# Second gate's products from three bfloat16 parts, two routings begun before a block end, and a rearranged last overflow tile in a fused attention and mixture-of-experts kernel

## What is computed

```python
def _moe_ref(x, w_skip, w_gate, w1, w2):          # first mixture
    do_compute = x @ w_skip > 0
    out = x.copy()
    xc = x[do_compute]
    logits = xc @ w_gate
    e_idx = np.argmax(logits, axis=1)
    gate_w = softmax(logits)[np.arange(len(xc)), e_idx]
    for e in range(E):
        mask = e_idx == e
        h = np.maximum(xc[mask] @ w1[e], 0.0)
        y[mask] = gate_w[mask, None] * (h @ w2[e])
    out[do_compute] = xc + y

def _moe2_ref(x, w_gate, w1, w2):                 # second mixture
    logits = x @ w_gate
    # (token, expert) pairs in falling order of their logit; a token goes to
    # the first expert that has room, and each expert takes N // E = 384
    for e in range(E):
        mask = assigned == e
        out[mask] = np.maximum(x[mask] @ w1[e], 0.0) @ w2[e]
```

## Time and profile before

| what | us |
|---|---|
| median of 3 runs | 808.35 |
| lowest and highest | 808.31, 808.92 |
| the profiled execution, whole | 809.03 |
| its span, first to last instruction | 807.3 |
| PE, DVE, ACT, POOL busy | 752.7, 536.9, 453.4, 165.3 |

### The profile page before, as it was taken

The page is one execution under the profiler, slowest core; times in us unless marked ns, Lnnn a source line. Parts: engine busy times, 40 slices in busy tenths (PEclk is TensorE's granted clock), DMA queues, the critical chain, the costliest instruction groups (busy, mean ns, idle before and its releaser), DMA issues. The chain is left out here.

```text
span 807.3 us, 15740 instructions
## 1 busy us (share of the span) xinstructions
PE 752.7 (93%) x5588; PEld 676.4 (84%) x5590; DVE 536.9 (67%) x1463; ACT 453.4 (56%) x919; POOL 165.3 (20%) x184
## 2 busy tenths in 40 slices
PE   2899999999869999999999929999999999999997
PEld 2899999999738998899988816888888888888895
DVE  6877878778388768775566557666676767675420
ACT  3899999989425545465454304555545454636360
POOL 8100000000030322213221101141414142323221
PEclk9999999999979999999999957999999999999999
DMA  8999989986265457634663007868676777769861
GB/s 180 218 214 251 227 195 251 217 227 177 107 180 196 156 216 250 217 129 165 228 233 122 18 2 248 201 198 202 204 188 209 186 220 187 220 180 303 225 126 44
DMA packets 64106, 151.65 MB, mean 188 GB/s; under 512 B 12294, under 2 KB 15750, under 8 KB 64016
## 3 DMA queue, kind: packets, MB, share of 16 engines
q1 hardware_dynamic: 52512, 114.77, 48.6%
q0 software_dynamic: 11504, 35.72, 18.3%
HBM read 118.84 MB, written 16.67 MB: 168 GB/s over the span
## 5 line engine op out<-in xcount | busy, mean ns | idle before, releaser
L1817 PE MATMUL r_ph<-r_xh,r_w1h 128*128 128x384 f32 x256 | 90.7, 354 | 0.0
L1817 PE MATMUL r_ph<-r_xh,r_w1l 128*128 128x384 f32 x256 | 86.2, 337 | 0.0
L1817 PE MATMUL r_ph<-r_xl,r_w1h 128*128 128x384 f32 x256 | 85.8, 335 | 0.0
L592 ACT ACTIVATE pr<-pr,nmx 128x232 f32<-128x232 f32 (+1 forms) x192 | 79.9, 467 | 4.1 <-DVE nmx L685 2.6
L1098 PE MATMUL m_ph<-m_xh,m_w1h 128*128 128x224 f32 x288 | 81.0, 281 | 0.1
L1252 ACT ACTIVATE m_hh<-m_ph 128x224 fp32r<-128x224 f32 (+1 forms) x72 | 25.1, 349 | 98.0 <-PE m_ph L1098 94.1
L1098 PE MATMUL m_ph<-m_xh,m_w1l 128*128 128x224 f32 x288 | 79.1, 275 | 0.0
L1098 PE MATMUL m_ph<-m_xl,m_w1h 128*128 128x224 f32 x288 | 79.0, 274 | 0.0
L685 DVE CUSTOM_DVE_ANT_0 pr<-sc,bias 128x232 f32<-128x232 f32 (+1 forms) x192 | 65.1, 375 | 19.4 <-PE sc L466 16.4
L599 ACT ACTIVATE prt<-tp 128x384 f32<-128x384 f32 (+1 forms) x128 | 65.3, 535 | 20.4 <-PE tp L478 17.0
L1831 PE MATMUL r_py<-r_w2h,r_hh 128*128 128x512 f32 x192 | 76.1, 397 | 0.0
(11 more groups left out here) (298 smaller groups left out, 1960.7 us busy)
## 6 DMA issues: line engine op xcount, KB each, us to landing
r_w<-moe_w SPq DMA_DIRECT2D x64, 512.0 KB, 5.1
m_w<-moe_w SPq DMA_DIRECT2D x36, 512.0 KB, 5.6
row_buf<-moe_w SPq DMA_DIRECT2D x9, 2048.0 KB, 8.7
r_w2l<-r_w POOLq DMA_DIRECT2D x32, 512.0 KB, 4.9
k_raw<-kI SPq DMA_DIRECT2D x64, 208.0 KB, 7.2
q_raw<-qT SPq DMA_DIRECT2D x64, 192.0 KB, 8.2
vo<-vL SPq DMA_DIRECT2D x16, 384.0 KB
x_rows<-row_buf SPq DMA_DIRECT2D x4, 1536.0 KB, 6.6
```

The lines of the kernel that those rows point to most:

```text
L592: nc.scalar.activation(pr[n % PRS][:, t, lo:CW], pr[n % PRS][:, t, lo:CW], ACT.Exp, bias=nmx[n % PRS][:, t:t + 1], scale=-1.0).then_inc(ex ...
L1817: last = nc.tensor.matmul(ph[m % 4][:, 0:CAP], w[:, c, m * P:(m + 1) * P], x[:, c, :], start=(c == 0 and a == 0), stop=(c == KC - 1 and a ...
```

## The change

1. **z of blocks 0 to 6 from bfloat16 parts.** ACT copies the transposed rows as bfloat16 (`y_parts[0]`), DVE subtracts that from the bank (`yt`), ACT takes the bfloat16 of the rest (`y_parts[1]`), DVE the rest of that (`y_parts[2]`). The gate's weights are split once, in `split_gate2`, four DVE operations put at the head of `count_extra`. The product takes each of the three parts of y with the 24 columns of the three parts of the gate: 24 bfloat16 products for a block instead of 8 float32 ones. DVE adds three columns for each logit (`tensor_reduce`) instead of copying. The z of block 7 and of overflow tiles stay in float32.
2. **Four steps instead of three**, behind chunks (1, 3, 4, 7), and (2, 3, 4, 5) in the overflow block. The product is the last step.
3. **`open_route`**: the first seven operations of `route` run on DVE at the end of the attention block, after `take_logits`. The semaphore `asked`, on which PE's counts waited, goes.
4. **Clearing**: `xg` is cleared by two ACT operations ahead of its w1 parts, not by POOL; POOL clears the ends of the three `y_parts` and waits for all six before it issues its first indirect DMA.
5. **`open_search`**: `bests`, `needs` and the first candidates (11 operations) run on DVE at the end of the first mixture's block.
6. **Overflow tile**: its four transposes go to four banks, without the wait for ACT between them. Four filler products follow the spreading of the marks, two follow the transpose of the limits.
7. **DVE's branches**: the code for n below 1 and over 1 comes before the code for n = 1, so that behind `put_z` none is left.

```diff
-BUSY1, BUSY2 = (18, 4, 3), (18, 4, 6)
+BUSY1, BUSY2, BUSY_END = (18, 4, 3), (18, 4, 6), (4, 2)
...
+                def open_route(link):
+                    by_expert = [P, E, NT]
+                    dve.wait_ge(filled, FILLS + 3)
+                    link(v.tensor_reduce(best1[:], logits[:, :, 0:E], AX.X, ALU.max))
+                    link(v.tensor_tensor(work1[:], logits[:, :, 0:E].rearrange("p t e -> p e t"), best1[:].unsqueeze(1).broadcast_to(by_expert), ALU.is_equal))
+                    link(v.tensor_scalar(live1[:], logits[:, :, E], 0.0, None, ALU.is_gt))
...
+                    link(v.tensor_tensor(hot1[:], work1[:], live1[:].unsqueeze(1).broadcast_to(by_expert), ALU.mult))
...
+                    dve.wait_ge(read, B)
+                    open_route(link)
...
-            Z_AT, OVER_AT = (2, 3, 5), 3
+            Z_AT, Z_LAST, OVER_AT = (1, 3, 4, 7), (2, 3, 4, 5), 3
...
+            def turned_rows(k, c):
+                return pt[c % 2][:, BLK:] if c < 2 or len(tiles(k)) == 2 else (py[1], ph[2])[c - 2][:, 0:P]
...
-                for s in range(2):
-                    g.memset(xg[s][:], 0.0).then_inc(cleared, 1)
                 g.memset(never[:], NO_ROW).then_inc(cleared, 1)
-                pool.wait_ge(cleared, 3)
+                for part in y_parts:
+                    g.memset(part[:, :, WIDE1:], 0.0).then_inc(cleared, 1)
+                pool.wait_ge(cleared, 6)
...
+                    elif i == 3 and in_parts(k):
+                        pe.wait_ge(yt_kept, kept_before(k) + 6)
+                        pe.wait_ge(yt_low, kept_before(k) + 6)
...
+                        for t in tiles(k):
+                            for c in range(KC):
+                                for a in range(3):
+                                    last = nc.tensor.matmul(pt[0][:, BLK + t * 3 * E:BLK + (t + 1) * 3 * E], y_parts[a][:, c, t * P:t * P + P],
+                                                            wg2_parts[:, c].rearrange("p a e -> p (a e)"), start=(c == 0 and a == 0), stop=(c == KC - 1 and a == 2))
+                        last.then_inc(z_done, 1)
...
-                pe.wait_ge(asked, 1)
...
                         nc.tensor.matmul(taken_p, spot_lane[:], spot_tile[:], start=True, stop=True).then_inc(taken_up, 1)
+                        keep_busy(BUSY_END[0], ph[3])
...
                         turn_limits()
-                    z_part(E, 0, 2)
+                        keep_busy(BUSY_END[1], ph[3])
+                    z_part(E, 0, 3)
...
+                    if i in (1, 2) and in_parts(k):
+                        two = slice(2 * i - 2, 2 * i)
+                        act.wait_ge(yt_low, kept_before(k) + 2 * i)
+                        nc.scalar.activation(y_parts[1][:, two, 0:WIDE1], yt[:, two, 0:WIDE1], ACT.Copy).then_inc(yt_kept, 1)
...
+                for s in range(2):
+                    nc.scalar.activation(xg[s][:].rearrange("p t d -> p (t d)"),
+                                         ones[:, 0:1].broadcast_to([P, TT1 * DM]), ACT.Copy, scale=0.0).then_inc(cleared, 1)
...
+                    if i < 2 and in_parts(k):
+                        for c in (2 * i, 2 * i + 1):
+                            dve.wait_ge(yt_kept, kept_before(k) + c + 1)
+                            v.tensor_tensor(yt[:, c, 0:WIDE1], pt[c % 2][:, BLK:BLK + WIDE1], y_parts[0][:, c, 0:WIDE1], ALU.subtract).then_inc(yt_low, 1)
+                    if i in (1, 2) and in_parts(k):
+                        two = slice(2 * i - 2, 2 * i)
+                        dve.wait_ge(yt_kept, kept_before(k) + 4 + i)
+                        v.tensor_tensor(y_parts[2][:, two, 0:WIDE1], yt[:, two, 0:WIDE1], y_parts[1][:, two, 0:WIDE1], ALU.subtract).then_inc(yt_low, 1)
...
+                def split_gate2():
+                    link(v.tensor_copy(wg2_parts[:, :, 0, :], wg2[:]))
+                    link(v.tensor_tensor(wg2_rest[:], wg2[:], wg2_parts[:, :, 0, :], ALU.subtract))
+                    link(v.tensor_copy(wg2_parts[:, :, 1, :], wg2_rest[:]))
+                    link(v.tensor_tensor(wg2_parts[:, :, 2, :], wg2_rest[:], wg2_parts[:, :, 1, :], ALU.subtract))
...
                 def count_extra():
+                    split_gate2()
...
+                with dve.If(n < 1):
+                    limits_of_all(Chain(dve, alone_chain))
+                with dve.If(n > 1):
...
                 with dve.If(n > 0):
-                    one_block(E, P)
                     with dve.If(n < 2):
+                        one_block(E, P)
...
                         put_z(alone)
+                        open_search(alone)
...
-                bests(logits2)
-                needs()
                 for r in range(TRIES):
                     attempt(0, r)
```

More of the change, by code:

```diff
@@ L804, in build @@
             yt = tb("yt", [P, KC, BLK])
+            y_parts = [tb(f"y_part{i}", [P, KC, BLK], BF16) for i in range(3)]
             zo = [tb(f"zo{s}", [P, TT1, E]) for s in range(2)]
@@ L1151, in over_table, with keep_busy @@
                     last.then_inc(over_placed, 1)
-                def keep_busy(times):
+                def keep_busy(times, bank=py[0]):
                     for i in range(times):
-                        nc.tensor.matmul(py[0][:], onesb1[:], busy[:, 0:512], start=True, stop=True)
-                pe.wait_ge(asked, 1)
+                        nc.tensor.matmul(bank[:], onesb1[:], busy[:, 0:512], start=True, stop=True)
                 flat = hot[:].rearrange("p e t -> p (e t)")
@@ L1277, in _ @@
                     one_block(E, P)
-                    for i in range(3):
+                    for i in range(4):
                         z_part(E, i)
@@ new lines, in limits_of_all, with more @@
+                def limits_of_all(alone):
+                    limit(alone)
+                    limit_all(alone)
+                    keep_limits(alone)
+                    open_search(alone)
+                def more(k):
+                    next_parts(k, 0, P)
+                    one_block(k, P)
+                    y_keep(k, 0)
+                    for i in range(4):
+                        z_part(k, 0, i)
+                with dve.If(n < 1):
+                    limits_of_all(Chain(dve, alone_chain))
@@ L1560, in _ @@
                         put_z(alone)
-                    with dve.If(n > 1):
-                        y_keep(E, 0)
-                        z_part(E, 0, 2)
-                def more(k):
-                    next_parts(k, 0, P)
-                    one_block(k, P)
-                    y_keep(k, 0)
-                    for i in range(3):
-                        z_part(k, 0, i)
-                further(dve, n, more)
-                for other in (n < 1, n > 1):
-                    with dve.If(other):
-                        alone = Chain(dve, alone_chain)
-                        limit(alone)
-                        limit_all(alone)
-                        keep_limits(alone)
+                        open_search(alone)
         late.close()
@@ L1607, in build @@
             masked, tie, ranks = (tb(x, shape) for x in ("masked", "tie", "ranks"))
-            work, hot, gt, taken = (tb(x, shape, BF16) for x in ("work", "hot", "over", "taken"))
+            work, hot, best, bestm, bestw, need, needc, scr8, span, candf = (
+                work2, hot2, best2, bestm2, bestw2, need2, needc2, scr2, span2, candf2)
+            gt, taken = (tb(x, shape, BF16) for x in ("over", "taken"))
             firstb = firstb1
-            best, bestm, cmp1, rank1, high = (tb(x, [P, NT]) for x in ("best", "bestm", "cmp1", "rank1", "high"))
-            bestw, cmpb, ours, mem, upto, low = (tb(x, [P, NT], BF16) for x in ("bestw", "cmpb", "ours", "mem", "upto", "low"))
+            cmp1, rank1, high = (tb(x, [P, NT]) for x in ("cmp1", "rank1", "high"))
+            cmpb, ours, mem, upto, low = (tb(x, [P, NT], BF16) for x in ("cmpb", "ours", "mem", "upto", "low"))
             cmp_ = tb("cmp", [P, NT, RADIX], BF16)
```

131 lines of the change are left out of this document (83 added, 48 removed).

## The result

The changed kernel takes 799.54 us in the median of four runs (799.36 to 799.70) beside 808.62 for the kernel before on the same chip: a ratio of 0.9888, 95% interval 0.9870 to 0.9905. That is 9.1 us less; the prediction said 10.05 less and 798.3, with a range of 796.3 to 803.0. In a later comparison the same kernel took 799.43 us (0.9892, 0.9878 to 0.9907). Its profiled execution took 799.55 us, 797.8 of them span.

What follows compares the result with a forecast made beforehand. PE was taken to bound the kernel, busy 752.7 of 807.3 us. Terms 5.95 - 0.3 + 0.6 + 3.8 = 10.05 us, off 808.35, gave 798.3 us; range 796.3 to 803.0.

Steps and rivals of the forecast that it cites:

- second boundary: Between the mixtures: DVE waits for PE and can work instead; moved search operations bring 2.4 us of the 3.8.
- z from parts: Blocks 0 to 6: z product takes 0.65 us instead of 1.50, 5.95 us less in all.
- The low end: Blocks 0 to 6: bfloat16 weights load as slowly as the earlier strided group, 7 x (1.5 - 1.7) = -1.4 us.
- Slack of DVE: Expert blocks: DVE's 2.6 us of new work a block costs nothing, covered by slacks of 4 and 5.3 us.
- third rival: Expert blocks: DVE becomes the bound in the h phase, making the kernel slower, 816.5 us; chance 0.05.
- split_gate2: Block 0's second tile: four DVE operations delay `y_keep`, PE waits 0.3 us once (0 to 0.8).
- The wait for the overflow list: Block 4: this wait stands a chunk earlier and costs nothing, at most 0.3 us.
- First boundary: Attention's end: seven routing operations ahead of the block end run undisturbed in 2.5 us, gaining 0.6 us.
- fifth rival: Both boundaries: the moved routings do nothing, so 2.4 + 0.6 us are missing, 801.3 us; chance 0.05.
- The held-up gather: First mixture's start: the w2 load holds up the first rows' gather, low end -1.0 us; a sign of error.
- Overflow tile: End of first mixture: four banks, full-clock z and placing, less fillers, give 1.4 us; 0.2 if the clock falls.
- fourth rival: Overflow tile's clock falls despite fillers, or PE's branch wait stays: 2.6 to 3.1 instead of 3.8, 799.3 us; chance 0.12.

Runs made afterwards that it cites:

- A: The changed kernel itself, with all parts of the change, against the kernel before: 799.54 us, ratio 0.9888.

## Why the prediction was right, point by point

The sum was 10.05 us, against 9.08 between the medians and 9.5 between the spans; each of its terms came within 0.15 us. Not all of them came for the reason given: the term of the second boundary, and with it part of the sum, was right by luck.

- **z from parts.** Right, and its size too: 0.65 us forecast for a product, 0.61 measured; 5.95 us forecast for seven blocks, 6.07 by the kernel with z in float32. The choice of the contiguous group of the earlier trace rows as the nearest row was right. The low end, the strided group, was a bound for something else: at a stride of 4 elements the product took 0.79.
- **Slack of DVE.** The result, no waits, was right; the working was not. The prediction took 4 us of slack for the last part of y and 5.3 for the low parts of h. In A the last part is done only 0.74 to 1.41 us before the product. With DVE's six operations doubled PE waits 0.25 us at the product, and with the same work in neighbouring chunks 1.0. The slack at the product was not "three chunks": the lumps, the copies by ACT and the low parts queued on DVE in between had used most of it. That the spacing (1, 3, 4, 7) was wide enough was thus closer than the prediction knew. The third rival (DVE the bound of h) stayed away: in no kernel do PE's waits in the expert blocks list a low part of h.
- **split_gate2.** Forecast 0.3 us, measured about 0.45 in block 1's h phase (a listed wait of 0.2 us and what it breaks). The wait for the overflow list cost nothing, as forecast.
- **First boundary.** The 0.6 us came (0.57 up to the counts; 0.54 up to the first h product, where executions differ by as much), but not by the move. The prediction took the 0.72 us of the block end as unchanged; behind the moved operations it lasted 0.95. The faster operations come from the clearing, and they would be as fast behind the block end. So the fifth rival is right for this boundary, and what is left is the change of the clearing. The held-up gather, which would have been a sign against the prediction, stayed away: from 236 us on PE's waits list 0.5 us for the gathered rows before, and none in A.
- **Overflow tile.** 1.4 forecast, 1.32 measured. The clock held to the end as said, and the fillers are what held it. The parts are joined: without fillers 0.87 us are lost, with two banks 0.84, of which the bank's wait is the 0.4 that the prediction put at 0.3 and the rest is the clock, which in that one execution fell just before the placing.
- **Second boundary.** 2.4 forecast, 2.25 measured, and the step that failed is its mechanism: "DVE waits for PE, and can work instead". DVE did become last. But PE's 3.2 us branch is gone in the changed program, so leaving the eleven operations where they were gives the same 3.98 us. The prediction held the branch for fixed and put its leaving into no case; its fourth rival has only the branch not moving with PE's work. The fifth rival's condition, that the moved operations do nothing, is met here too, but its price of 2.4 us is not paid, since the gain came by other ways: about 1.05 us because PE's long branch went, and about 1.2 because DVE lost its branches behind `put_z` (five in the trace, four by the prediction). The kernels with z in float32 show that with such a branch the move is worth 3.2 us. By the Trainium skill (Runtime: NRT & Kernel Launch, Instruction fetch mechanics) a taken branch out of the fetched window waits for a DMA. The instruction loads inside or just ahead of PE's branches of 0.77 to 3.8 us agree; the page gives no length to reckon with.
- **What no step had.** The attention ends 0.57 us later in the profile, with PE's first branch 0.75 us longer.

How long a branch waits goes with when its load of instructions begins. Why a program has that load earlier or later stays open: it is not the count of PE's instructions alone, and mostly not chance, for the same program gave 7.22 and 7.36 us at the first branch, and 1.06 and 0.77 at the other.

## What to carry to other kernels

Work put on an engine with idle time is free only if its pieces lie where that engine has its gaps: the same 2.6 us a block cost nothing at chunks (1, 3, 4, 7) and 1.6 us a block at (2, 3, 4, 5), so a sum of idle time says whether there is room, and only the chain from one piece to the next says whether it comes in time. Here "cost nothing" means no wait: a slack of 0.6 to 1.3 us was left. When work is moved across a meeting of engines, ask first who comes last and whether that lateness belongs to work or to a branch, which another edit of the same change can take away. In a short chain at the end of a stage, look at when PE's clock falls: fillers moved that from 2.8 or 3.3 us behind the start of the mark product to 4.3 or later, and in the one execution in which the chain was 0.4 us longer it lost 0.4 us more by the clock.

## What the runs showed of the hardware

- The length of a taken branch on PE depends on the program around it: one line 0.36, 0.64, 0.77, 1.06, 1.42, 3.6 and 3.8 us in kernels that differ elsewhere. At that boundary it ends 1.34 to 1.38 us after the 16 KB load of instructions that lies in it or just ahead of it (1.50 in the kernel without fillers).
- From the end of the last engine's drain to DVE's next operation a block end took 0.28 us at the second boundary. At the first it took 0.67 us behind DVE's drain before, and 0.68 in A.
- bfloat16 weights 4 elements apart: 24 products in 0.79 us against 0.61 contiguous. Writing bfloat16 with that stride costs ACT and DVE about double: 736 ns against 353 for 224 columns (ACT), 1186 against 617 for 448 (DVE). Reading it costs DVE nothing to speak of: 387 against 382 for 224.
- DVE's operation on 24 columns takes 0.18 us beside ACT's clearing of `xg`, and 0.93 beside POOL's.
